# Attention's result turned in 32 by 32 blocks on VectorE and laid out by transfers through memory

## What is computed

```python
def _attn_ref(x, weight_gen):          # x (4, 4096, 192), weight_gen (4, 4096, 8, 7)
    w = np.exp(weight_gen - max over the taps); w = w / (sum of w + 1e-09)
    x_pad = six zero tokens ahead of x
    out[b, s, h, g] = sum over k of w[b, s, h, k] * x_pad[b, s + k, h, g]   # 8 heads of 24

def _moe_ref(x, w_in, w_out):          # x (16384, 192), w_in (192, 2048), w_out (2048, 192)
    h = x @ w_in
    relu6 = np.clip(h + 3.0, 0.0, 6.0)
    g = h * relu6 / 6.0
    return (g @ w_out).astype(np.float32)
```

## Time and profile before

| | us |
|---|---|
| median of 3 runs | 1191.66 (1189.92 to 1194.54) |
| the profiled execution, its own time | 1187.49 |
| its span | 1185.5 |
| TensorE busy | 1151.4 |
| VectorE busy | 818.9 |
| GpSimd busy | 690.7 |
| ScalarE busy | 662.0 |

### The profile page before, as it was taken

How to read it: one execution, slowest core, us unless ns; L and a number is a source line. 1 busy time by engine, 2 the same in 40 slices (tenths; PEclk the granted TensorE clock), 3 DMA queues, 4 the chain that set the end, 5 groups by cost and what they waited for, 6 DMA issues and landing times.

```text
span 1185.5 us, 33838 instructions
## 1 busy us (share of the span) xinstructions
PE 1151.4 (97%) x13696; PEld 1070.8 (90%) x13696; DVE 818.9 (69%) x1362; ACT 662.0 (56%) x1269; POOL 690.7 (58%) x455
## 2 busy tenths in 40 slices
PE   1899999999999999999999999999999999999998
PEld 1799999999999999999999999999999999999997
DVE  7966767667676767667677676776767667676664
ACT  3555555555555555555555555555556555555554
POOL 7794581927739195590936729186490945819200
PEclk9999999999999999999999999999999999999999
DMA  6101010010100101001010100101001010100000
GB/s 185 48 23 61 0 47 33 21 60 21 46 13 21 60 21 60 0 21 60 21 60 21 46 13 21 60 21 60 0 21 60 21 60 6 46 28 13 15 15 14
DMA packets 12077, 42.18 MB, mean 36 GB/s; under 512 B 1183, under 2 KB 5279, under 8 KB 10139
## 3 DMA queue, kind: packets, MB, share of 16 engines
q1 hardware_dynamic: 12059, 41.93, 10.0%
HBM read 29.34 MB, written 12.58 MB: 35 GB/s over the span
## 4 chain that ended last, share of the span: by engine, by line
PE 96%; DVE 2%; POOL 1%; issue 0%; DMA 0%; ACT 0%; DVEq 0%; ACTq 0%
PE sums L548 34%; PE work L512 16%; PE sums L551 15%; PE work L526 14%; PE work L527 9%; PE work L513 7%; PE work L477 1%; PE work L464 0%; DVE w_out L419 0%; POOL pool_acc L166 0%; POOL pool_prod L164 0%; DVE w_in L413 0%; DMA w_raw<-weight_gen_dram 0%; PE work L463 0%; DVE g_lo L362 0%
## 5 line engine op out<-in xcount | busy, mean ns | idle before, releaser
L548 PE MATMUL sums<-w_out,g_hi 64*128 64x384 f32 x4096 | 631.0, 354 | 3.9 <-DVE g_lo L362 3.3
L551 PE MATMUL sums<-w_out,g_lo 64*128 64x192 f32 x4096 | 536.1, 247 | 0.0
L357 DVE SCALAR_TENSOR_TENSOR work<-relu,work 128x512 f32<-128x512 f32 x512 | 331.3, 693 | 280.9 <-ACT relu L261 279.7
L261 ACT ACTIVATE relu<-work 128x512 f32<-128x512 f32 x512 | 279.4, 601 | 349.6 <-PE work L527 346.5
L548 PEld LDWEIGHTS sums<-w_out,g_hi 64*128 64x128 f32 x4096 | 410.2, 184 | 23.3 <-issue 3.5
L551 PEld LDWEIGHTS sums<-w_out,g_lo 64*128 64x128 f32 x4096 | 415.7, 187 | 0.0
L266 ACT CAST g_hi<-work 128x512 fp32r<-128x512 f32 x512 | 300.6, 587 | 76.7 <-DVE work L357 74.0
L362 DVE TENSOR_TENSOR g_lo<-work,g_hi 128x512 fp32r<-128x512 f32 x512 | 330.1, 686 | 14.1
L166 POOL TENSOR_TENSOR pool_acc<-pool_acc,pool_prod 128x768 f32<-128x768 f32 (+1 forms) x160 | 295.5, 1847 | 0.0
L159 POOL TENSOR_TENSOR pool_acc<-x_in,w_soft 128x768 f32<-128x768 f32 (+1 forms) x32 | 50.0, 1563 | 410.8 <-DVE w_soft L351 403.8
L164 POOL TENSOR_TENSOR pool_prod<-x_in,w_soft 128x768 f32<-128x768 f32 (+1 forms) x160 | 248.7, 1555 | 0.0
(11 more groups left out here) (47 smaller groups left out, 954.3 us busy)
## 6 DMA issues: line engine op xcount, KB each, us to landing
x_in<-x_dram SPq DMA_DIRECT2D x15, 1344.0 KB, 6.0
out_dram<-out_stage SPq DMA_DIRECT2D x32, 384.0 KB, 2.8
w_raw<-weight_gen_dram SPq DMA_DIRECT2D x16, 224.0 KB, 3.0
w_out_raw<-moe_w_out_dram SPq DMA_DIRECT2D x1, 1152.0 KB, 13.8
x_in<-x_dram SPq DMA_DIRECT2D x1, 768.0 KB, 4.7
w_in_raw<-moe_w_in_dram SPq DMA_DIRECT2D x1, 768.0 KB, 9.1
w_in_raw<-moe_w_in_dram SPq DMA_DIRECT2D x2, 384.0 KB, 10.6
w_out_raw<-moe_w_out_dram SPq DMA_DIRECT2D x1, 384.0 KB, 6.8
```

Of the source, the lines that this page charges most:

```text
L261: nc.scalar.activation(t.relu[:, m % 2, :], t.work[m % BANKS][:], ACT.Relu, bias=3.0).then_inc(s.relu_ready, 1)
L357: nc.vector.scalar_tensor_tensor(bank[:], t.relu[:, m % 2, :], 6.0, bank[:], ALU.min, ALU.mult).then_inc(s.gated, 1)
L548: nc.tensor.matmul(t.sums[n][:, 0:2 * D], t.g_hi[rows, m % G_SLOTS, n * P:(n + 1) * P], t.w_out[rows, j, :], start=(j == 0 and part == 0), ...
L551: ins = nc.tensor.matmul(t.sums[n][:, D:2 * D], t.g_lo[rows, m % G_SLOTS, n * P:(n + 1) * P], t.w_out[rows, j, 0:D], start=False, stop=las ...
```

## The change

The pairs' layout in the partitions changes: partition 32b + r now holds run r of batch b. The address pattern of a load counts 4 batches, then 32 runs, then the stretch. The halo of the first pair is loaded by four DMAs, one a batch, of 31 runs each.

The transposes on TensorE stay for the very first half only. For every other half VectorE turns 32 by 32 blocks within each group of 32 partitions (`turn`: two instructions, 128x512 and 128x256, SBUF to SBUF, into `blocks`). SP writes `blocks` to a DRAM tensor `columns` (`spread`, one DMA of 384 KB) and reads it back in eight DMAs (`gather`, 32 partitions each, pieces of 512 bytes) into SBUF tensors `x_a` and `x_b`. From these `x_hi` and `x_lo` make `xt_a` and `xt_b`, where before they read PSUM.

The duos of transposes go, and a pair has 16 duos. In pairs 1 to 15 VectorE turns half 1 behind duo 2 and the next pair's half 0 behind duo 11, and the splits stand behind duos 5 and 14. In pair 0 it is duos 4 and 12, and 6 and 14. TensorE waits for the split in the first fill of duos 8 and 16 (`fill_first`). A store becomes four DMAs of 32 partitions, in pieces of 768 bytes but for the first. `g_hi` and `g_lo` have 8 slots, where they had 6.

```diff
-X0_DMAS = 3
+X0_DMAS = 1 + B
...
-G_SLOTS = 6
+G_SLOTS = 8
+ROUND = 2 * TILES
...
+SECOND_TURN_AT, SECOND_SPLIT_AT = (4, 2), (6, 5)
+FIRST_TURN_AT, FIRST_SPLIT_AT = (12, 11), (14, 14)
...
-        return bass.AP(a.tensor, start, [[TOKENS * per_token, r1 - r0], [S * per_token, B], [1, count]])
+    def in_dram(a, per_token, start, count):
+
+        return bass.AP(a.tensor, start, [[S * per_token, B], [TOKENS * per_token, RUNS], [1, count]])
...
-    for r0, r1 in ((1, RUNS // 2 + 1), (RUNS // 2 + 1, RUNS)):
-        sp.dma_start(t.x_in[B * r0:B * r1, 0:HALO * D],
-                     in_dram(dram.x, D, (TOKENS * r0 - HALO) * D, HALO * D, r0, r1)).then_inc(s.x_loaded, 16)
+    for b in range(B):
+        sp.dma_start(t.x_in[RUNS * b + 1:RUNS * (b + 1), 0:HALO * D],
+                     bass.AP(dram.x.tensor, b * S * D + (TOKENS - HALO) * D,
+                             [[TOKENS * D, RUNS - 1], [1, HALO * D]])).then_inc(s.x_loaded, 16)
...
+    def spread(q, half):
+
+        sp.wait_ge(s.turned_blocks, 2 * (2 * q + half + 1))
+        sp.dma_start(dram.columns, t.blocks[:]).then_inc(s.columns_written, 16)
+
+    def gather(q, half):
+
+
+        sp.wait_ge(s.columns_written, 16 * (2 * q + half))
+        for e in range(DA // BLOCK):
+            sp.dma_start(t.x_a[BLOCK * e:BLOCK * (e + 1), :],
+                         bass.AP(dram.columns.tensor, e * P, [[COLUMNS, BLOCK], [BLOCK * COLUMNS, B], [1, P]])
+                         ).then_inc(s.columns_loaded, 16)
...
+    load_next_weights(0)
+    spread(0, 1)
+    gather(0, 1)
+    load_next_x(0)
+    store(0, 0, by_run=True)
+    spread(1, 0)
+    gather(1, 0)
+    load_next_weights(1)
+    load_next_x(1)
+    store(0, 1)
+    with sp.Fori(1, PAIRS - 2) as q:
+        spread(q, 1)
+        gather(q, 1)
         store(q, 0)
-        load_next(q + 1)
+        spread(q + 1, 0)
+        gather(q + 1, 0)
+        load_next_weights(q + 1)
+        load_next_x(q + 1)
         store(q, 1)
...
-            pool.wait_ge(s.transposed_a, 2 * q - 1 + half)
-            pool.wait_ge(s.transposed_b, 2 * q - 1 + half)
+            pool.wait_ge(s.turned_blocks, 2 * (2 * q + half - 1))
...
+    def x_hi(q, half):
+        act.wait_ge(s.columns_loaded, GATHER * (2 * q + half))
+        x_hi_a(half, t.x_a)
+        x_hi_b(half, t.x_b)
...
+    def turn(q, half, first=False):
+
+        dve.wait_ge(s.attn_ready, 2 * (2 * q + half))
+        if not first:
+            dve.wait_ge(s.columns_loaded, GATHER * (2 * q + half - 1))
+        for attn, c0, c1 in ((t.attn_a, 0, DA), (t.attn_b, DA, D)):
+            nc.vector.transpose(t.blocks[:, c0 // BLOCK:c1 // BLOCK, :].rearrange("p e (t r) -> p t e r", r=BLOCK),
+                                attn[:, half, :].rearrange("p (t e c) -> p t e c", t=GT, c=BLOCK)
+                                ).then_inc(s.turned_blocks, 1)
...
+    def x_lo(q, half):
+        dve.wait_ge(s.xt_hi_ready, inputs_split(q, half))
+        x_lo_a(half, t.x_a)
+        x_lo_b(half, t.x_b)
...
+        if d == SECOND_TURN_AT[not first]:
+            turn(q, 1, first)
+        if d == SECOND_SPLIT_AT[not first]:
+            x_lo(q, 1)
...
+        if d == FIRST_TURN_AT[not first]:
+            turn(q + 1, 0)
+        if d == FIRST_SPLIT_AT[not first]:
+            x_lo(q + 1, 0)
...
+    def fill_first(q, d):
+
+        if d % HALF_DUOS == 0:
+            pe.wait_ge(s.xt_lo_ready, inputs_split(q, d // HALF_DUOS))
```

More of the change, by code:

```diff
@@ L80, in turns_before, with inputs_split @@
     return 1 + 2 * (DUOS - 1) * q + 2 * (d - FIRST_DUO) + second_fill - ended
-def skipped(m, last):
-    return last and (m >= ROUND or (m >= SLOTS and not is_tile(m)))
 def tiles_done(q, m):
-    return 2 * TILES * q + sum(is_tile(i) for i in range(m + 1))
+    return ROUND * q + m + 1
 def duos_filled(q, d):
[L95 to L106, removed]
+    return DUOS * q + d + 1
+def inputs_split(q, half):
+    return SPLIT_PARTS * (2 * q + half + 1)
 def x_loads(q):
@@ new lines, in store @@
+    def store(q, half, by_run=False):
+        sp.wait_ge(s.out_staged, 2 * GT * q + GT * (half + 1))
+        for i in range(GT):
+            start = q * PAIR_X + half * GT * D
+            if by_run:
+                to = bass.AP(dram.out.tensor, start + i * S * D, [[TOKENS * D, RUNS], [1, GT * D]])
+            else:
+                to = bass.AP(dram.out.tensor, start + i * D, [[TOKENS * D, RUNS], [S * D, B], [1, D]])
+            sp.dma_start(to, t.out_stage[BLOCK * i:BLOCK * (i + 1), half, :]).then_inc(s.stored[half], 16)
@@ L282, in evacuate, with duo @@
                           1.0 / 6.0).then_inc(s.main_staged, 1)
-    def duo(q, d, last=False):
+    def duo(q, d, first=False, last=False):
         if d == HALF_DUOS + 1:
@@ L317, in scalar_program @@
     act.wait_ge(s.transposed_a, 1)
-    x_hi(0, TA, t.work[BANKS - 2])
+    x_hi_a(0, t.work[BANKS - 2])
     act.wait_ge(s.transposed_b, 1)
-    x_hi(0, TB, t.work[BANKS - 1])
+    x_hi_b(0, t.work[BANKS - 1])
+    act.sem_inc(s.turned_blocks, 2)
     w_out_hi(1)
-    for d in range(FIRST_DUO):
-        duo(0, d)
-    with act.Fori(0, PAIRS - 1) as q:
+    for d in range(FIRST_DUO + DUOS):
+        duo(0, d, first=True)
+    with act.Fori(1, PAIRS - 1) as q:
         for d in range(FIRST_DUO, FIRST_DUO + DUOS):
@@ L426, in vector_program @@
     dve.wait_ge(s.x_loaded, x_loads(0))
-    dve.wait_ge(s.halo_zeroed, 1)
+    dve.wait_ge(s.halo_zeroed, B)
     attend(nc.vector, t, t.dve_prod, t.dve_acc, 0, 0, SPLIT, s.dve_step, 0, s.attn0_ready)
     w_in_lo(0)
-    for i, what in enumerate((TA, TB)):
-        dve.wait_ge(s.xt_hi_ready, 2 * i + 1)
-        x_lo(0, what, t.work[BANKS - 2 + i])
+    dve.wait_ge(s.xt_hi_ready, 1)
+    x_lo_a(0, t.work[BANKS - 2])
+    dve.wait_ge(s.xt_hi_ready, SPLIT_PARTS)
+    x_lo_b(0, t.work[BANKS - 1])
     w_in_lo(1)
     w_out_lo(0)
-    duo(0, 0)
+    duo(0, 0, first=True)
     w_out_lo(1)
-    for d in range(1, FIRST_DUO):
-        duo(0, d)
-    with dve.Fori(0, PAIRS - 1) as q:
+    for d in range(1, FIRST_DUO + DUOS):
+        duo(0, d, first=True)
+    with dve.Fori(1, PAIRS - 1) as q:
         for d in range(FIRST_DUO, FIRST_DUO + DUOS):
```

194 lines of the change are left out of this document (86 added, 108 removed).

## The result

The changed kernel takes 1336.14 us (median of 4 runs, 1332.44 to 1337.9); the kernel before, beside it on the same chip, 1190.79 us. The ratio is 1.121, with a 95% interval of 1.1175 to 1.1245. The forecast was 1273 us with a range of 1225 to 1310: the sign was right, and the loss is 145 us where 81 were forecast.

What follows compares the result with a forecast made beforehand. TensorE, 96% of the span, was taken as the bound. Transposes -22, split stop +57, loads +24, pair 0 +20 and end +2 gave +81 on 1187.5, so 1268.5 us, or 1273 as median; range 1225 to 1310.

Steps and rivals of the forecast that it cites:

- the clock: TensorE behind each stop at duo 16: the sum booked no loss for a fall from 2.4 to 1.2 GHz.
- The sum: Whole kernel: -22 + 57 + 24 + 20 + 2 = +81 us on the profiled 1187.5; chance 0.57.
- Rival 1: TensorE's clock falls at every pair's stop too: 14 x 2.4 = 34 us more, 1307 us; chance 0.11.
- The way through memory: Columns written and read back: 9.7 us within about 11.5, so hidden in pairs 1 to 15, 2 us in hand.
- The loads on few engines: x_in and weights on 4 engines, each halo load on one: attention starts at 33.5 us, 24 us lost.
- The transposes: 31 groups leave TensorE at 0.7 us each: 22 us gained.
- The stop behind duo 14: Split held up by GpSimd: TensorE stands 4.1 us before duo 16, 14 times, 57 us lost.
- Pair 0: Late x_in delays turn and split before duo 16: 17 us, plus 3 for slow fills, 20 us lost.
- The end: The last store becomes four issues at 0.62 us: 2 us lost.
- 16 engines: Rival 2: all 16 engines carry the loads, start loses 1.5 us, pair 0 9.5: 1240 us; chance 0.16.
- Split free: Rival 3: loads on few engines, but the split behind duo 14 isn't held up: 1212 us; chance 0.07.
- Neither: Rival 4: split not held up and loads keep their rate: 1182 us, 0.8% faster; chance 0.09.

Runs made afterwards that it cites:

- after: The changed kernel itself as profiled, with no further edit: 1337.9 us in that execution, against 1187.5 us for the kernel before.
- pause: Changed kernel, with GpSimd waiting ahead of the last product of its second half until the split behind duo 14 is done: 1338.3 us.
- loads16: Changed kernel with halo16's edit, and every load of x_in and window weights made one transfer a batch, first count 32: 1281.7 us.
- both: Changed kernel with the edits of loads16 and pause together: 1193.8 us, ratio 1.005 to the kernel before.
- early: As both, but duo 14's split stands ahead of its g_hi and g_lo, and GpSimd pauses one product sooner: 1189.3 us, ratio 1.001.
- halo16: Changed kernel with each of the first pair's four halo loads made two, of 16 and 15 rows: 1331.8 us.

## Why the prediction was wrong

The forecast had 81 us lost; the profiled executions differ by 150.4. The steps that failed stand first.

- **The step that failed most: the clock, put at nothing.** The sum let TensorE go on at the fast clock behind each stop. Rival 1, given 0.11, came true beside the forecast: the 14 duos behind the stops take 30 us more than at the fast clock, 2.1 us each for the rival's price of 2.4. Without these 30 us the sum comes to some 1306 us, inside the range. It should have been part of the forecast: the earlier trace rows show a fast clock behind 2.5 us of idling, the stop was to be 4.1 us, and no row spoke for its surviving that. I set the chance by the lack of a row, not by the nearest one.
- **The way through memory: wrong, some 14 us, and more lay hidden.** "Hidden, with 2 us in hand" was worked out without the queue (and 3 x 4.42 less 1 is 12.3, not 11.5). Undisturbed, the last read has landed 7.2 us after the write was issued at 684.50, for the 9.7 forecast, so some 5 us were in hand. Behind the `x_in` load the write alone takes 9.0 us, for 2.9, and the last read lands 13.9 us after 643.23. The text said that the write queues there and uses up the 2 us, and let it end at that. In after this costs 7.5 us in duo 7 of pair 1 and 1.0 to 1.9 us in five of pairs 2 to 14 (0.5 on average), only because the stop covers the rest; pause shows the whole of it.
- **The loads on few engines: right in kind** (share 0.27 for four engines, 0.07 for one), late by 8 us at the start (41.74 for 33.5). The weights and `x_in` are through near 14 us, some 2 us late. The halo rows then have one engine at 25 GB/s, but from 32 us on the layer's weights use all 16 engines, this one too (share 0.78 to 1.09), and the trace's packets of the halo fall from 5 or 6 a us to 2 or 3. The sum counted the first engine's own 825 KB and not what was issued behind it. "27 GB/s each" made the loop's load 15 us. At the 59 GB/s of its window it takes 23 by estimate, and the write behind it landed 24.5 us after the load's issue.
- **The transposes: mis-sized.** 22 us were written, 31 groups x 0.7. The working took two duos behind the group at 4.42 us each, but the loss is 0.48 us a group over the whole half (0.96 a pair), 15 us; and nothing of it is the transposes' own.
- **The stop behind duo 14: right**, in place, cause and nearly in size: 62.2 us in the 14 waits of pairs 1 to 14, for 57. The turn-taking of the earlier trace rows repeats in every pair. That the pair shown has 4.17 us for 4.1 is in part luck, since they spread from 3.3 to 6.1. The turns were sized well too: 0.70 and 0.40 us, 1.1 a half for 1.0, and no TensorE idle behind them in the loop.
- **Pair 0: right, 19.8 us for 20,** by TensorE's first fills (its two groups of transposes, 1 us, are in the 19.8 and not in the 20). GpSimd waits 31.79 us for `x_in`, and TensorE stops 11.99 and 4.97 us. The chain forecast for it is the one seen, with the slow load in it and the clock low behind both stops. What the forecast lacked is pair 1, 14.6 us for the 2.7 of any pair: its columns are late as well.
- **The end: 2 us forecast and 2.0 measured, by luck.** From the last matmul to the end of the span it is 5.06 us, 4.49 before, so the four issues cost 0.6. The rest is mostly the slow clock behind the last stop.
- **The sum.** A pair of the loop costs 6.3 us, by TensorE's first fills, for 2.7: 2.1 by the clock, 0.5 by the late columns, 0.44 by the transposes, 0.6 by the stop.
- **The rivals.** 16 engines, 1240: loads16 is that case, 1281.7; it lacked the clock as well. Split free, 1212: pause is that case, 1338.3, where the rival had put nothing behind the stop. Neither, 1182: both and early, 1193.8 and 1189.3.

## What to carry to other kernels

Two waits that end near each other are one wait in the trace: before a gain is booked for taking the later one away, ask what is ready when without it, and take both away in one run. A stop longer than any that the trace shows at the fast clock is to be priced with the slow clock behind it. A transfer's time isn't its own: what was issued ahead of it on the same engines counts first, and a pattern that begins with a small count keeps those few engines busy for long. What a removed instruction costs is read from the gap between its neighbours, not from its duration.

## What the runs showed of the hardware

- Four DMA engines that write rows of 10.5 KB to four 32-partition groups carry 16 GB/s each, with rows of 6 KB 24 in after and 18 in halo16; 16 engines that write 32 partitions 15, one alone 25, and 16 over all partitions 23 to 26.
- A queue's issue can stall: with four halo loads on one engine SyncE needs 14.95 us to issue them and 5.36 us for the next load (after), where eight loads dealt to more engines take 3.60 us (halo16).

```profile
2.13 14.95 SPq L177 DMA_DIRECT2D x_in<-x_dram  x4
17.13 5.36 SPq L183 DMA_DIRECT2D w_in_raw<-moe_w_in_dram  x1
```
```profile
2.14 3.60 SPq L178 DMA_DIRECT2D x_in<-x_dram  x8
```

- Issues of small transfers are cheap: eight reads of columns in 3.6 us, 0.45 each, for the 0.62 of the earlier trace rows. They land in 1.9 us (the page of after, median), though cut into pieces of 512 bytes.
- A 4.17 us stop of TensorE had the clock at 1.2 GHz before it ended, and it came back 5.4 us after work began again. Behind a stop of 4.19 us it fell 0.9 us after work had begun and was low for 3.4 us.
- VectorE and GpSimd, each with instructions that read two SBUF operands, take turns one instruction at a time: three subtractions take 5.6 us beside GpSimd and 1.6 alone.
